# A tile's row number read into a register without a range check, and a planner told of it

## The reference

```python
f = lower_bound + (1 - lower_bound) * sigmoid(f_logit);  i = 1 - f
for t in range(S):
    h = f[:, t] * h + i[:, t] * x[:, t]
    y[:, t] = h
...
expert_idx = argmax(cosine(x, expert_emb) / tau)      # x is y, as (20224, 256)
for e in range(E):
    h = np.maximum(x[mask] @ w1[e], 0.0)              # 256 -> 1024
    out[mask] = gate_w[mask, None] * (h @ w2[e])      # 1024 -> 256
```

## Time and profile before

| | us |
|---|---|
| median of 3 runs | 586.08 |
| lowest and highest | 584.51, 588.92 |
| the profiled execution | 582.69 |
| its span, from the first to the last instruction | 580.8 |

### The profile page before, as it was taken

One profiled execution on the slowest core, in us unless ns is written; L12 is line 12 of the kernel. 1 busy time (PEld: TensorE's weight loads), 2 busy tenths in 40 slices (PEclk: granted clock), 3 DMA queues, 4 the chain that ended last, 5 costly groups with the idle time before them and its releaser, 6 DMA issues.

```text
span 580.8 us, 12467 instructions
## 1 busy us (share of the span) xinstructions
PE 486.7 (84%) x4100; PEld 389.6 (67%) x4100; DVE 360.9 (62%) x1042; ACT 321.4 (55%) x546; POOL 339.0 (58%) x408
## 2 busy tenths in 40 slices
PE   7898978787989688888888887888877898898895
PEld 4566654556767576658655677777766787787795
DVE  7979988677778677786867663434443444343452
ACT  4878887756677666767766433323333333233442
POOL 6264766466565565555656556556656665565555
PEclk7999999899999898989989989989999999898998
DMA  8999999999999998999846446433433325444431
GB/s 252 302 328 292 321 309 227 147 257 252 269 201 257 262 237 195 235 219 226 213 120 118 98 100 145 112 102 97 110 100 94 87 77 112 106 111 111 109 50 47
DMA packets 127586, 101.80 MB, mean 175 GB/s; under 512 B 104532, under 2 KB 106591, under 8 KB 127520
## 3 DMA queue, kind: packets, MB, share of 16 engines
q1 hardware_dynamic: 111104, 60.70, 42.4%
q0 software_dynamic: 16416, 40.27, 28.7%
HBM read 58.38 MB, written 34.01 MB: 159 GB/s over the span
## 4 chain that ended last, share of the span: by engine, by line
PE 62%; ACT 10%; DVE 7%; issue 7%; DMA 6%; another core or an unknown queue 5%; SPq 1%; POOL 1%; ACTq 0%; POOLq 0%; DVEq 0%
PE bank L1320 23%; PE bank L1365 23%; PE bank L788 4%; PE bank L754 4%; PE bank L908 4%; ACT hT L1338 4%; DMA xm<-XsScratch 3%; DMA xin<-in_x_dram 2%; DVE hb L812 2%; ACT fg L771 2%; DVE bank L796 1%; ACT th L765 1%; DVE hT L1343 1%; PE bank L498 1%
## 5 line engine op out<-in xcount | busy, mean ns | idle before, releaser
L1390 POOL DMA_INDIRECT out_dram<-osb,xm x166 | 164.8, 993 | 120.4 <-issue 35.0
L1365 PE MATMUL bank<-wall,hT 128*128 x1328 | 178.9, 278 | 45.5 <-ACT hT L1338 36.7
L1072 POOL DMA_INDIRECT XsScratch<-Yt,sli x158 | 152.9, 968 | 97.7 <-issue 27.1
L1320 PE MATMUL bank<-ys,wall 128*128 128x256 bf16 x1328 | 179.9, 282 | 6.8 <-issue 3.3
L1343 DVE TENSOR_SCALAR hT<-bank 128x512 bf16<-128x512 f32 x166 | 112.5, 686 | 113.6 <-PE bank L1320 68.5
L1365 PEld LDWEIGHTS bank<-wall,hT 128*128 128x128 bf16 x1328 | 126.4, 99 | 77.3 <-ACT hT L1338 45.6
L1338 ACT ACTIVATE hT<-bank 128x512 bf16<-128x512 f32 x166 | 97.4, 596 | 141.4 <-PE bank L1320 92.2
L1320 PEld LDWEIGHTS bank<-ys,wall 128*128 x1328 | 153.0, 145 | 17.4 <-issue 6.4
L812 DVE TENSOR_TENSOR_SCAN hb<-fg,hb,bank 128x512 f32<-128x512 f32 (+4 forms) x78 | 96.2, 1238 | 0.1
L1384 DVE TENSOR_SCALAR osb<-bank,xm 128x256 f32<-128x256 f32 x83 | 39.9, 481 | 64.1 <-ACT osb L1380 37.7
L1380 ACT ACTIVATE osb<-bank,xm 128x256 f32<-128x256 f32 x83 | 39.3, 473 | 59.1 <-issue 25.8
(11 more groups left out here) (128 smaller groups left out, 306.4 us busy)
## 6 DMA issues: line engine op xcount, KB each, us to landing
fin<-in_f_logit_dram SPq DMA_DIRECT2D x39, 512.0 KB
xin<-in_x_dram SPq DMA_DIRECT2D x39, 512.0 KB
wall<-in_moe_w_dram POOLq DMA_DIRECT2D x16, 512.0 KB, 10.7
out_dram<-osb,xm POOLq DMA_INDIRECT x166
XsScratch<-Yt,sli POOLq DMA_INDIRECT x158
ys<-XsScratch SPq DMA_TRANSPOSE x83
xm<-XsScratch SPq DMA_DIRECT2D x83, 2.0 KB
XsScratch<-nulr SPq DMA_DIRECT2D x8, 136.0 KB
```

The costliest lines, as they stand in the source:

```text
L1072: lambda e, j=o + j, i=o + k_ * 4 + b: e.indirect_dma_start(out=Xs[:, :], out_offset=bass.IndirectOffsetOnAxis(ap=sli[y][:, j : j + 1], axis=0
L1320: i = e.matmul(bank[hh[f // 2].b][:, (f % 2) * T : (f % 2 + 1) * T], wall[:, bass.ds(a1[j][(4 * mp + f) * DT + kt] - WA - WREV, 2 * FT * P ...
L1365: i = e.matmul(po(s), hT[qh][:, kf, s * P : (s + 1) * P], wall[:, bass.ds(a2[j][kf] - WA, 2 * D)].bitcast(BF16), start=(kf == 0 and (s == ...
L1390: lambda e, s=s: e.indirect_dma_start(out=out[:, :], out_offset=bass.IndirectOffsetOnAxis(ap=xm[qx][:, s, 1:2], axis=0), in_=osb[qo][:, s, :],
```

## The change

`ld` used `value_load` with bounds, which reads the register and writes a check that the value lies between 0 and `NULLROW`. It now allocates a register by name, reads it with a plain `load`, and turns it into an expression with `snap`, to which the bounds are told. The expression serves the same two DMAs. Beside it the planned cost of `ld` goes from 2050 to 1750 ns, that of `ldm` from 650 to 570.

```diff
             def ld(e):
-                r = e.value_load(tbl[u][j : j + 1, 0:1], min_val=0, max_val=NULLROW)
-                evl[j] = r
+                r = reg(e, f"row{j}")
+                e.load(r, tbl[u][j : j + 1, 0:1])
+                r = evl[j] = e.snap(r, donate=True, min_val=0, max_val=NULLROW)
                 return e.dma_start_transpose(
                     ys[qy][:], Xs[bass.ds(r, T), 0:P].bitcast(BF16)
                 )
...
-            lo = op("sp", ld, 2050, r=rd, w=[("ys", qy)], dma=f"xs{qy}", nbytes=290000)
-            op("sp", ldm, 650, r=rd, w=[("xm", qx)], dma=f"xm{qx}", nbytes=66000, order=[lo])
+            lo = op("sp", ld, 1750, r=rd, w=[("ys", qy)], dma=f"xs{qy}", nbytes=290000)
+            op("sp", ldm, 570, r=rd, w=[("xm", qx)], dma=f"xm{qx}", nbytes=66000, order=[lo])
```

## The result

| | before | changed |
|---|---|---|
| median, us (22 runs each) | 586.12 | 581.44 |
| lowest and highest, us | 580.32, 593.38 | 578.02, 584.36 |
| ratio to before | | 0.9941 (95% interval 0.9919 to 0.9962) |
| profiled execution and its span, us | 582.69, 580.8 | 583.08, 581.2 |

The ratio leaves out executions in which the chip ran disturbed, so it is not the quotient of the medians; 0.0059 of 586 us are 3.5 us (2.2 to 4.7). The two profiled executions are of one length: the one of before was 3.4 us shorter than its median, the one of after 1.6 us longer. So the two traces tell what sits where, but a difference of their totals tells nothing.

What follows compares the result with a forecast made beforehand. TensorE, busy 84% of 580.8 us, was taken to bound the kernel, with SyncE's time mostly hidden. Profiled 582.69 - 0.5 (earlier loads) + 0 (plan) = 582.2 us, or 585.6 on the median's scale; predicted 585.5, range 576 to 593.5.

Steps and rivals of the forecast that it cites:

- the likeliest case: Freed SyncE time stays hidden, its waits grow, the order shuffles by a few microseconds: 585.6 us, 582 to 589; chance 0.56.
- What is removed: On SyncE, each of 83 tiles loses the range check's two instructions: about 0.3 us a tile, 24.9 us in all.
- The rival that the check stays: The snap with bounds writes the assert again, SyncE keeps its rows, only the plan changes: 586 us; chance 0.03.
- The cover in the tile stage: Loads run up to six buffers ahead; SyncE's 34.8 us of waits for a free `ys` buffer absorb the freed time.
- The cover in the mixed stage: Recurrence and tiles mixed: cover thinner only at the first tiles; two loads 0.3 us sooner gain at most 0.6, taken 0.5.
- The first sign of being wrong: Forecast is wrong if a tile's load proves to end TensorE's waits where the view names ScalarE; no size given.
- The Trainium skill's rule: Sequencer time saved on starting a transfer is usually small beside the transfer; by it the gain is 0, not 0.5 us.
- The plan: SyncE's planned tile cost falls from 2700 to 2320 ns, reordering the mixed stage; 9.8 us less to 7.4 more, taken 0.
- The size of the shuffle: If the six mixed-stage windows are shuffled rather than moved one way, their spread adds up to 2.7 us.
- The denser stage: From 85 to 325 us, earlier loads fill TensorE's holes at the best window's pace: 9.8 us less, 576 us; chance 0.22.
- Early products ahead of their rows: First tiles' products planned before their rows land, so TensorE waits: three more such waits, 8.4 us, 594 us; chance 0.16.

Runs made afterwards that it cites:

- twice the time: Kernel before, in its order, with the checked register read done twice for tiles 35 to 82 only: ratio 1.0036 (0.9997 to 1.0075).
- The 21 us put in there: Kernel before, in its order, with the checked register read done twice for tiles 0 to 34 only: ratio 1.0078 (1.0048 to 1.0107).
- four plans: Plain load with planned costs 2050/650, 1900/610, 1750/570 and 1600/530 ns, against the kernel before: ratios 0.9984, 1.0003, 0.9943 and 1.0029.
- the same half of this change: New planned costs (1750 and 570 ns) with the checked load kept, against the kernel before, run twice: ratios 0.9996 and 0.9954.

## Why the prediction was right, and where its sum was off

The forecast was 585.5 us, with "within 1%" at 0.56. Measured were 581.44 us and 0.59% less: the range and the class hold, and the time lies 0.6 us under the 582 to 589 us that the likeliest case was given. The sign was not called with any confidence, and the number itself was close to no change: 0.6 us less were forecast, 3.5 us came. So the range and the mechanism in the tile stage hold, and the gain's size was not foreseen.

- *What is removed.* Right. The check was 0.3 us of a tile, it is gone, the register load stayed at 283 ns, the MOVE stayed. The rival that the check stays is out.
- *The cover in the tile stage.* Right as far as it was tested: L1321 has 0.9 us of waits after 345 us, where the forecast said none, and the wait for a buffer, into which the freed time was to go, grew by 10.9 us (25 us were its upper end). That twice the time costs nothing there is not shown; the run came out between nothing and 0.75%.
- *The cover in the mixed stage.* Wrong. The step took SyncE's 34.8 us of waits for a buffer, a sum over the run, as cover for all tiles but the first two. By stretch, those waits are none in 85 to 165 us, where SyncE waits 6.4 us in all. The 21 us put in there came out at 22%. By the same share, taking 35 x 0.3 = 10.5 us out would be worth 2.3 us; the term of the sum was 0.5 us. Measured for it were 0.9 +- 1.6 us, so 2.3 us lies inside, and so do 0.5 us and nothing. That the price of more and the gain of less are the same is not shown; the load of tile 20, 8.9 us later with more and at most 1.6 us earlier with less, speaks against it.
- *The first sign of being wrong.* The forecast named one: a tile's load that proves to end TensorE's wait where the view names ScalarE's L924. It came true: the wait before tile 1's first product is put down to the `ys` DMA in all six other profiles with the order of before, 2.9 to 7.7 us. It costs the forecast little, since the sum had let that wait count as one that a load could end.
- *The Trainium skill's rule.* The Trainium skill ("DMA: Bandwidth & Descriptors", Issuing engines are not separate DMA queues) says that starting DMAs from several engines at once saves only the sequencer's time to start them, usually small beside the DMA itself. For the one load of the earlier trace rows the trace agrees: 0.42 us of issue, 16.56 us to land. But the time here is register work ahead of an issue, on a queue that is full: 0.6 us more of it on each of 35 tiles gave 4.6 us. So that rule was no reason for zero.
- *The plan.* The size of the shuffle was right: 2.7 us estimated from the spread of the windows, 2.1 us among four plans. The middle of zero was the honest value, and this draw came out at -1.8 +- 1.3 us. That the plan could let `xm` slip ahead of the transposes was seen, and happened; that it mattered was not so.
- *The rivals.* The denser stage asked for 34.2 us of TensorE in each window; it is 33.76, so it did not decide. But what came out is that rival's effect in small: 30 matmuls more from 85 to 345 us, and 3.5 us of its full price of 9.8. That early loads filling TensorE's holes did it is not shown. Early products ahead of their rows did not happen: the early wait of L1320 fell. It was the wrong way round: the order of before had that trouble.

What stays open: which exchange in the order makes the 1.8 us and the matmuls gained by 345 us, and whether the plain load in the old order gains anything. The times of both are at or under what these runs resolve.

## What to carry to other kernels

Ask for the cover of an engine's time by stretch, not by its sum over the run: a queue with 35 us of such waits in a run may have none in the stretch where it matters, and adding work to it in one stretch at a time shows in which stretch it costs. To compare two orders by their traces, count what is done by a given time; busy time hides it when the clock differs. When an edit also changes the costs of a planner, run the edit and the costs apart, and try a neighbour or two of the costs, since a new order is a draw from a spread (here about 2 us) that says little on whether the costs are better. An effect of half a per cent wants a second measurement: the same half of this change came out at 0.04% and then at 0.46%.

## What was unexpected

One pair of transposes of the recurrence held SyncE for 16.04 us, where the pairs behind it take 1.0 to 3.4 us, most of them 2.5 to 2.6; a small `xm` load took 16.56 us to land; both with the DMA engines at a share of 1.14. In the other six profiles with the order of before the same pair took 9.3 to 13.1 us. So in that stretch a DMA's issue is no short instruction, and what stands behind it in the queue waits as long. With the pair before it (5.59 us) it fills 21.6 of the 30 us from 85 us on; after 120 us ordinary issues fill SyncE.
